# Recurrent attention and two dense layers on one core: sums and state update on column halves, the result moved by DMA

## The reference

```python
def _attn_ref(r, k, v, w, u):            # (4, 8, 768, 48) each, u (8, 48)
    for t in range(S):
        cur = u * k_t (outer) v_t
        y[t] = r_t @ (state + cur)
        state = w_t[:, None] * state + k_t (outer) v_t
x = attn_out.transpose(0, 2, 1, 3).reshape(3072, 384)
x = (sigmoid(x @ w_gate) * (x @ w_val)) @ w_out      # d_ff 1536
h = x @ w_in                                          # d_ff 2048
out = elu(h) @ w2_out
```

## Time and profile before

| | us |
|---|---|
| median of 3 runs | 1180.27 (1179.73 to 1181.82) |
| the profiled execution's own time | 1178.09 |
| its span | 1176.4 |
| TensorE busy | 1142.6 (97%) |
| VectorE busy | 606.0 (52%) |
| ScalarE busy | 476.5 (41%) |
| GpSimd busy | 329.5 (28%) |

### The profile page before, as it was taken

One profiled execution on the slowest core, in us unless ns is written; L12 is line 12 of the kernel. 1 busy time (PEld: TensorE's weight loads), 2 busy tenths in 40 slices (PEclk: granted clock), 3 DMA queues, 4 the chain that ended last, 5 costly groups with the idle time before them and its releaser, 6 DMA issues.

```text
span 1176.4 us, 17093 instructions
## 1 busy us (share of the span) xinstructions
PE 1142.6 (97%) x6660; PEld 1018.9 (87%) x6660; DVE 606.0 (52%) x925; ACT 476.5 (41%) x919; POOL 329.5 (28%) x292
## 2 busy tenths in 40 slices
PE   6798899999999999999999999999999999999998
PEld 5788899888888888888888888789999998999998
DVE  6887667646555555655565533353434333343433
ACT  2545343332333333323332323364545444454543
POOL 7434456454435442635273500000000000000000
PEclk8999999999999999999999999999999999999999
DMA  7536044040404040404140031220101001010000
GB/s 127 102 100 123 14 69 62 21 61 7 68 27 62 8 67 29 61 7 61 35 61 8 1 121 57 65 81 1 54 1 54 1 1 55 1 54 1 27 1 28
DMA packets 155856, 52.42 MB, mean 45 GB/s; under 512 B 126720, under 2 KB 153472, under 8 KB 155776
## 3 DMA queue, kind: packets, MB, share of 16 engines
q1 hardware_dynamic: 155776, 51.33, 21.8%
HBM read 41.88 MB, written 9.44 MB: 44 GB/s over the span
## 4 chain that ended last, share of the span: by engine, by line
PE 89%; DVE 5%; ACT 2%; issue 2%; SPq 1%; DMA 1%; DVEq 0%
PE ps L620 24%; PE ps L653 17%; PE ps L645 17%; PE ps L629 12%; PE ps L566 10%; PE ps L581 3%; PE ps L556 3%; PE ps L594 2%; PE ps L586 2%; DVE RKW L821 1%; DVE WS L920 1%; DVE A L853 1%; PE ps L536 1%; ACT RKW L676 1%; SPq L281 1%
## 5 line engine op out<-in xcount | busy, mean ns | idle before, releaser
L620 PE MATMUL ps<-xh,WS 128*128 128x512 f32 (+1 forms) x1008 | 258.8, 374 | 2.1 <-DVE xl L895 1.0
L676 ACT ACTIVATE hh<-work 128x512 fp32r<-128x512 f32 (+1 forms) x180 | 108.9, 605 | 282.4 <-DVE work L910 197.7
L653 PE MATMUL ps<-WS,hh 128*128 128x384 f32 x768 | 198.1, 339 | 0.5 <-DVE hl L899 0.5
L620 PEld LDWEIGHTS ps<-xh,WS 128*128 128x128 f32 x1008 | 168.9, 190 | 27.6 <-DVE work L910 1.4
L474 POOL TENSOR_TENSOR RKW<-RKW,WL 128x256 f32<-128x256 f32 x144 | 145.7, 1013 | 147.4 <-PE ps L566 147.3
L899 DVE TENSOR_TENSOR hl<-work,hh 128x512 fp32r<-128x512 f32 (+1 forms) x180 | 131.7, 732 | 91.6 <-ACT hh L676 91.0
L629 PE MATMUL ps<-hh,WS 128*128 128x512 f32 (+1 forms) x504 | 168.4, 379 | 6.3 <-DVE hl L899 6.2
L566 PEld LDWEIGHTS ps<-RKW 128*128 128x128 f32 x1152 | 152.8, 197 | 23.4 <-DVE RKW L821 13.6
L566 PE MATMUL ps<-RKW 128*128 128x128 f32 x1152 | 158.2, 282 | 12.1 <-DVE RKW L821 11.7
L645 PE MATMUL ps<-xh,WS 128*128 128x512 f32 x576 | 164.2, 397 | 0.0
L937 DVE SCALAR_TENSOR_TENSOR work<-work,ps 128x512 f32<-128x512 f32 x96 | 66.0, 688 | 169.3 <-ACT work L769 169.3
(11 more groups left out here) (70 smaller groups left out, 1298.2 us busy)
## 6 DMA issues: line engine op xcount, KB each, us to landing
nat<-in_w_dram SPq DMA_DIRECT2D x24, 192.0 KB, 3.7
nat<-in_k_dram SPq DMA_DIRECT2D x24, 192.0 KB, 4.8
nat<-in_r_dram SPq DMA_DIRECT2D x24, 192.0 KB, 5.3
V<-in_v_dram SPq DMA_DIRECT2D x24, 192.0 KB, 4.8
x_scratch<-work SPq DMA_DIRECT2D x12, 384.0 KB, 3.3
nat<-x_scratch SPq DMA_DIRECT2D x6, 768.0 KB, 6.0
out_dram<-Yt SPq DMA_DIRECT2D x5, 768.0 KB, 4.3
RKW<-in_moe_w_in_dram SPq DMA_DIRECT2D x16, 192.0 KB, 2.4
```

The costliest lines, as they stand in the source:

```text
L620: last = mm(ps[:, VAL if val else GATE, t], gate_w(a, val, j, c), xp[b][:, c, t], start=(i == 0 and c == 0), stop=(i == 2 and c == KC - 1))
L653: last = mm(ps[:, ACC2 + b, 0:HD], hp[ap][:, j % 2, b * P:(b + 1) * P], down2_w(wp, j), start=(j == 0 and i == 0), stop=(j == F2 - 1 and i ...
L676: return nc.scalar.activation(o, i, ACT.Copy)
```

## The change

- `Y` on column halves: v (48 columns) is loaded as weights and `A` (128 columns) streams; then the state (48 columns) is loaded and `RP` (128 columns) streams. Head e = 0 writes PSUM partitions 0 to 47, e = 1 writes 64 to 111. The result stands transposed, one pair on 128 columns. `S` likewise: 48 columns of k are loaded, 48 of v stream.
- The diagonal terms go into `A`: POOL makes r'k, rk and u.r.k (at L1 to L3), DVE sums them to `dots`, mixes even and odd rows to `near`, and copies `near` into `A` through a new mask at `KT`. `AV`, its load, three POOL operations per half and the DVE add are gone.
- ACT copies the result of each part to `yT`; SP moves it to `xs` by 10 DMAs per half (`move_y`). ACT and DVE make `xh` and `xl` from `xs` (`split_y`), before the `LATE` row. The transposes are gone.
- The shares of `spread` and the room are new; four stages of q = 1 are issued before the first dense step.

```diff
@@ spread, PROGRAM @@
+    EVEN = {**{(name, b): 1 for name in STAGES for b in range(U)},
+            ("KT", 1): 2}
+    SHORT = {**{(name, b): x for name, x in (("Tw", 2), ("Tk", 2), ("Tr", 2), ("L1", 5), ("L2", 5), ("L3", 5), ("L4", 4),
+                                             ("L5", 2.5), ("L6", 2.5)) for b in range(U)},
+             ("KT", 0): 1, ("KT", 1): 4, ("Y", 0): 0, ("Y", 1): 0, ("S", 0): 0, ("S", 1): 2}
-    PROGRAM = STREAM[:STREAM.index(("x", 0)) + 1]
+    LEAD = len(PARTS[0]) + 4
+    PROGRAM = USES[:LEAD] + [("x", 0)]
...
+        room = len(THIRDS[m]) - (9 if len(SETS[m][1]) == 2 else 14)
...
+            PROGRAM += [("x", m + 1)] + LATE[m]
@@ sync @@
+            def move_y(q):
+                hf, m = q % HALF, set_of(q)
+                sp.wait_ge(a_y, 2 * (q + 1))
...
+                for head in range(H):
+                    g, e = head // 2, head % 2
+                    lo, end = head * D, (head + 1) * D
+                    for f in range(lo, end, 16):
+                        if f > lo and f % P:
+                            continue
+                        stop = min(end, (f // P + 1) * P)
+                        sp.dma_start(xs[f % P:f % P + stop - f, f // P, hf * TH:(hf + 1) * TH].rearrange("f (b t) -> f b t", b=U),
+                                     yT[e * HP + f - lo:e * HP + stop - lo, :, g * P:(g + 1) * P]).then_inc(xs_loaded, 16)
...
-            load_shift(v, 0)
...
+                    if phase["a", q, "S", 1] == m:
+                        move_y(q)
@@ gpsimd @@
-            TERMS = {("Tr", 1): "rk", ("L1", 1): "u", ("L2", 1): "rk'", ("L5", 1): "v'", ("L6", 1): "v", ("KT", 0): "sum"}
+            TERMS = {("L1", 1): "r'k", ("L2", 1): "rk", ("L3", 1): "u"}
@@ tensor @@
-            def transpose_x(m):
...
-                            mm(y[:, p, e, :], A[:, g, e, :], V[:, hf, g, e, :],
+                    pe.wait_ge(d_diag, 2 * q + b + 1)
+                            mm(bank[e * HP:e * HP + D, p * P:(p + 1) * P], V[:, hf, g, e, :], A[:, g, e, :],
...
-                        last = mm(y[:, p].rearrange("p e d -> p (e d)"), RP[:, g, :],
-                                  ST[:, hf, g].rearrange("p e d -> p (e d)"),
+                        for e in range(2):
+                            last = mm(bank[e * HP:e * HP + D, p * P:(p + 1) * P], ST[:, hf, g, e, :], RP[:, g, :],
...
-                        last = mm(bank[:, p * 2 * D:(p + 1) * 2 * D], KM[:, g, :],
-                                  V[:, hf, g].rearrange("p e d -> p (e d)"), start=True, stop=True)
+                        for e in range(2):
+                            last = mm(bank[e * HP:e * HP + D, p * D:(p + 1) * D], KM[:, g, e * HP:e * HP + D],
+                                      V[:, hf, g, e, :], start=True, stop=True)
@@ scalar @@
+                elif name == "Y":
+                    act.wait_ge(s_att, count("a", q, name, b))
+                    if b == 0:
+                        wait(act, xs_loaded, 16 * MOVES * q)
+                    copy(yT[:, b, :], ps[:, bank_of("a", q, name, b), :]).then_inc(a_y, 1)
+            def split_y(m):
+                act.wait_ge(xs_loaded, 16 * MOVES * (HALF * n + halves[-1] + 1))
+                if m >= HALF:
+                    act.wait_ge(s_v, F1 * m)
                 for c in range(KC):
-                    copy(xh[:, c, t], ps[:, bank_of("x", m, c), t]).then_inc(a_xhi, 1)
+                    copy(xh[:, c, t], xs[:, c, t]).then_inc(a_xhi, 1)
@@ vector @@
-                elif name == "Y":
-                    tt(Yt[:, hf * G + b * PR:hf * G + (b + 1) * PR, :, :], AV[:, pairs],
...
+                elif name == "KT":
+                    dve.wait_ge(a_score, level(q, NL - NM - 1, b, NL - NM))
+                    dve.wait_ge(d_near, 2 * (q + 1))
+                    nc.vector.copy_predicated(
+                        A[:, pairs].rearrange("p g e (i j) -> p (g e) i j", j=2),
+                        masks[:, 0, :].bitcast(I32).unsqueeze(1).unsqueeze(3).to_broadcast([P, 2 * PR, i, 2]),
+                        near[:, 2 * b * PR:2 * (b + 1) * PR].unsqueeze(2).to_broadcast([P, 2 * PR, i, 2])).then_inc(d_diag, 1)
```

More of the change, by code:

```diff
@@ L85, in build, with spread @@
     LATE = [[("d", m, "o", j, i) for j in (F1 - 2, F1 - 1) for i in range(3)] for m in range(NS)]
-    def spread(dense, parts, room, share=None):
-        share = [share[part[2]] if share and part[0] == "a" else 1 for part in parts]
+    EVEN = {**{(name, b): 1 for name in STAGES for b in range(U)},
[3 more added lines that the diff above has]
+             ("KT", 0): 1, ("KT", 1): 4, ("Y", 0): 0, ("Y", 1): 0, ("S", 0): 0, ("S", 1): 2}
+    def spread(dense, parts, room, share):
+        before = [sum(share[part[2:]] for part in parts[:x]) for x in range(len(parts) + 1)]
         steps = []
@@ L92, in spread @@
             steps.append(third)
-            steps += [parts[s] for s in range(len(parts)) if int(sum(share[:s]) * room / sum(share)) == i]
+            steps += [part for x, part in enumerate(parts) if int(before[x] * room / before[-1]) == i]
         return steps
-    SHARE = {"Tw": 2, "Tk": 2, "Tr": 2, "L1": 5, "L2": 5, "L3": 5, "L4": 4, "L5": 2.5, "L6": 2.5, "KT": 1, "Y": 0.5, "S": 0.5}
-    PROGRAM = STREAM[:STREAM.index(("x", 0)) + 1]
-    done = len(PROGRAM)
+    LEAD = len(PARTS[0]) + 4
+    PROGRAM = USES[:LEAD] + [("x", 0)]
+    done = LEAD
     phase = {}
     for m in range(NS):
[L104 to L108, removed]
-        else:
-            PROGRAM += spread(THIRDS[m], beside, len(THIRDS[m]) - 1, SHARE) + LATE[m]
-    assert done == len(STREAM)
+        room = len(THIRDS[m]) - (9 if len(SETS[m][1]) == 2 else 14)
+        if m + 1 < NS:
+            until = len(PARTS[0]) * (HALF * SETS[m + 1][0] + SETS[m + 1][1][-1] + 1) + MORE.get(m, 0)
+            beside = USES[done:until]
+            done = until
+            phase.update({step: m for step in beside})
+            if m in MORE:
+                cut = len(beside) - MORE[m]
+                PROGRAM += spread(THIRDS[m], beside[:cut], room, SHORT)[:len(THIRDS[m]) + cut]
+                rest = beside[cut:]
+                tail = PROGRAM[-(len(THIRDS[m]) - room):]
+                PROGRAM = PROGRAM[:-len(tail)]
+                for x, step in enumerate(tail):
+                    PROGRAM.append(step)
+                    PROGRAM += rest[x * len(rest) // len(tail):(x + 1) * len(rest) // len(tail)]
+            else:
+                PROGRAM += spread(THIRDS[m], beside, room, EVEN if len(SETS[m][1]) == 2 else SHORT)
+            PROGRAM += [("x", m + 1)] + LATE[m]
+        else:
+            PROGRAM += THIRDS[m] + LATE[m]
+    assert done == len(USES) and len(set(PROGRAM)) == len(PROGRAM) == len(USES) + NS + sum(len(x) for x in THIRDS + LATE)
     N1 = 3 * F1
@@ L497, in attention @@
                     term(q, TERMS[name, b])
-            for step in STREAM:
-                if step[0] == "a":
-                    attention(*step[1:])
+            for step in USES:
+                attention(*step[1:])
         @block.tensor
@@ L789, in _ @@
                 elif step[0] == "x":
[L790 removed]
+                    split_y(step[1])
                 else:
```

226 lines of the change are left out of this document (97 added, 129 removed).

## The result

The changed kernel took 1159.91 us (median of 4 executions, 1158.80 to 1166.42), against 1180.0 before in the same session. The ratio is 0.9839, 95% interval 0.9801 to 0.9877. The profiled execution took 1160.17 us with a span of 1158.5. The forecast was 1159. That the two agree is in large part luck, as the stages show.

What follows compares the result with a forecast made beforehand. TensorE, busy 97% of the span, was taken as the bound. Full sets −19.2, m = 1 −3.8, m = 0 −1.5, lead +3.5 sum to −21.0: 1178.1 to 1157.1 profiled, 2.2 below the median, so forecast 1159 us; range 1142 to 1190.

Steps and rivals of the forecast that it cites:

- the prediction's largest bet: In Y, two column halves stream side by side, two records sharing some 106 ns: 1.7 us a part, gain 0.9.
- the first rival: In Y's 32 records, halves don't run side by side, 106 ns each instead of 53: 1196 us in all; chance 0.18.
- Y and S: Parts on column halves in TensorE's stream: Y 1.7 us, a gain of 0.9; S 0.67 us, a gain of 0.14.
- Going in and out: Switching between dense steps and column halves costs 0.08 us more for each of 48 Y and S parts.
- high end: Upper bound for switching in and out of halves: one whole record more on each side, 0.2 us a part.
- A full set: Sets with TensorE never idle: Y and S 4.2, transposes 1.2, less 0.6 for switching: −4.8 us, 120.3 to 115.5.
- The lead: Before the first dense step: masked copy, Y and transfer make it 4.0 later, transposes −1.4, clock 0.9: +3.5 us, bounds 0 and +9.
- an issue ... I take 0.37: Each of the ten DMA issues moving a half's result takes 0.37 us, 3.7 in all; rows gave 0.34 to 0.65.
- The landing: Arrival of the moved x after the DMA issues: 2.5 us taken, between 1.9 and 6.0 us in the rows.
- m = 0 and m = 1: First two sets, where stages also wait for other engines: savings of 2.6 and 3.8 us, counted as 1.5 and 3.8.
- Late transfer: Move of x: hidden in full sets, up to 1 us in m = 1; as rival, slow landing and issues, 1177 us, chance 0.08.
- The signs: Wrong if sets shrink under 3 us or m = 0, 1 idle grows over 5.4; xl wait absent from m = 2, dense start about 51.

Runs made afterwards that it cites:

- experiment 1: Changed kernel with both heads of a pair written to the same column half in Y and S, against the kernel before: 1208.36 us, ratio 1.0263.
- experiment 4: Changed kernel with Y0, Y1, S0, S1 of a half in a row in full sets too, against the kernel before: 1150.62 us, ratio 0.9777.
- kernel before with 1184 bytes: Kernel before with 1184 unused bytes a partition ahead of xh, giving working tensors the addresses of the kernel after: 1167.43 us, ratio 0.9896.
- experiment 5: Changed kernel with one DMA per half for ten, x misplaced: 1152.64 us; in another run, five of the first half's ten issued by ACT: 1161.69 us.
- experiment 6: Changed kernel with the last ten dense weights' loads issued between the DMAs of q = 2's loads, against the kernel before: 1154.97 us, ratio 0.98.
- experiment 2: Unused bytes ahead of xh: kernel before with 32, 1152, 1184 bytes took 1174.85, 1172.46, 1167.43 us; kernel after with 32 took 1169.9 us.

## Why the prediction was right, and where it wasn't

The direction held, and so did the mechanism in its main part: TensorE bounds the sets, and halves run side by side. The statement that `Y` and `S` pay for weight columns holds for the kernel before, where 48 streamed columns are free, but it is not what the gain comes from: without overlap a part of either costs no less than before (experiment 1). The gain hangs on the overlap, the prediction's largest bet. Experiment 1 shows that the first rival was the real alternative: it gave 1208 where 1196 had been predicted for it.

The agreement of the total is a sum of errors that cancel. In the span, the stages that the change touches gave 8.5 us where 21.0 were forecast, and 9.4 us came from stages to which the forecast gave nothing. The 2.2 us that it added to get from the profiled execution to the median weren't there either: the profiled one, forecast at 1157.1, took 1160.17, and the median was 1159.91.

- *Y and S.* Predicted 1.7 and 0.67 us a part, measured 1.88 and 0.49. Sum of both 2.37, forecast 2.37. For `S` the forecast took no overlap; without it experiment 1 has 0.85.
- *Going in and out.* Predicted 0.08 us a part more, "as much again". Measured 0.10 in and 0.04 more than another stage out, 0.14. Eight parts: 0.5 us a set that the forecast missed. The "high end", 0.2, held it. Here the Trainium skill's rule on draining ("TensorEngine Tiling (Array Packing)", Key Properties) pointed the right way: experiment 4 shows that each stop saved gives 0.35 us, 0.10 of it on the way in.
- *A full set.* Predicted −4.8. With the place of the operands taken out (118.9 to 115.4, kernel before with 1184 bytes against kernel after) it is −3.5. Of the missing 1.3 us, 0.5 are going in and out, and 0.75 the two waits that the forecast did not have, one of them where the transposes had stood. The prediction took 120.3 us as the length of a set from one window; from start to start it was 119.6, so its 115.5 for the set after was met by 115.3 for the wrong reason. The first full set, m = 2, gave only 2.6 us, since the clock fell behind the late x.
- *The lead.* Predicted +3.5 us, measured +10.4, above the +9 that was given as its bound. This is the step that failed. Like with like, the first dense step was forecast at 50.9 us and came at 57.2, 6.3 us later. Most of that, 3.4 us, is the term "an issue ... I take 0.37": it was 0.71 in the lead, above the 0.65 at the top of the range given, and 0.65 at m = 2, so ten cost 7.1 us instead of 3.7. Experiment 5 shows that 5.4 us of the lead hang on it. Another 2.9 us are `Y` and the `Y` part behind it at 3.4 us and 3.0 instead of 1.7 each, at a granted clock of 0.59, since TensorE had waited 3.6 us: the forecast had put a price on the clock behind the second wait only. Next, `Y` began at 39.8, not 38.8: DVE's pair ahead of the masked copy took 2.02 us, not 1, and the masked copy, priced at the 0.905 us of one of 512 elements, has 1024 and took 1.29. The landing, forecast at 2.5 us behind the last issue, took 2.0 from that issue's start and gave back 1.1.
- *m = 0 and m = 1.* Predicted −1.5 and −3.8, measured −0.8 and −2.8, and −1.9 and −2.6 against the kernel before with 1184 bytes. In m = 0 the loss is a wait for a weight load behind other loads on SP's queue, worth 4.6 us (experiment 6). The forecast also split m = 0 from m = 1 at the wrong time, which changes no number of its sum. It looked at SP's queue for what stands before the move, not for what stands before the weights.
- *Late transfer.* "In m = 1 up to 1 us may show": 2.15 us of wait showed at the start of m = 2. With one DMA (experiment 5) m = 1 is 1.5 us shorter, and m = 2, behind which the clock no longer falls, 1.6. In the full sets after that it stayed hidden.
- *Untouched stages.* Predicted nothing, measured −9.4 us in m = 6 and layer 2, and 0.7 in each full set. Not in any rival. Of the 20 us of the result, 12 are the place of the operands (experiment 2, kernel before with the same addresses), and the change as written is worth the other 7 to 8. That the forecast of 21 met 20 is luck.
- *The signs.* Sets shrank by more than the 3 us named as the limit, and idle time in m = 0 and m = 1 grew by 4.3 us, less than the 5.4 named. But the wait for `xl` was not absent at m = 2, it was 7.7 us and not 5 at the end of the lead, and the dense start was not at 51.

## What to carry to other kernels

Where a small matmul pays as much for 48 streamed columns as for 128, loading 48 and streaming 128 on two column halves nearly halves the price of a record, here from 108 to 59 ns, but only if neighbours in the stream use different halves; keep such stages in one run, since each stop among full-width matmuls cost 0.35 us here. Before crediting a change with its gain, compare the stages that it doesn't touch: here more than half of the gain was the place of tensors in memory, which one unused tensor shows. A transfer cut into ten pieces is priced by ten issues on its queue, a second queue has a price on its engine, and what stands ahead on a queue can make a load late that the kernel needs sooner.

## What the runs showed of the hardware that was not expected

A matmul of 512 columns of float32r took 235 ns in one layout of the working tensors and 229 in another, and of 384 columns 176 and 173 (medians from start to start in layer 2). A shift by 32 bytes was worth 2.4 to 5.4 us of layer 2. Without overlap, a float32 record of 48 loaded and 128 streamed columns took 109 ns, one of 48 and 48 took 45 (experiment 1), and one of 128 and 48 took 112 (kernel before). SBUF to SBUF DMAs of up to 48 partitions with two runs of 512 bytes each followed one another on SP at 0.65 us (at m = 2), though a load of 128 rows from memory took 0.34. A masked copy of 128x1024 took 1.29 us in the lead and 1.69 us in the mean over the kernel:

```profile
L898 DVE COPY_PREDICATED A<-masks,near 128x1024 f32<-128x1024 int32 x24 | 39.4, 1685 | 0.2
```
